# The second expert layer with its first product turned round, weights loaded for every tile, and another ending

## The chip, the cores and the metric

The kernel runs on one core of a Trainium2 chip. The metric is the device time of one execution in microseconds (us). A run of the profiler gives the trace of one execution, in which each engine's instructions stand with their starts and lengths.

## The reference

Three stages follow one another. All data are 32-bit floats.

```python
# 1: attention over 4 x 8 heads, 768 positions, 64 features: a band of +-15 keys, and block summaries of 32 keys
# 2: experts with a capacity: 3072 rows of 512, 8 experts with 384 rows each
h = np.maximum(x[mask] @ w1[e], 0.0);  out[mask] = h @ w2[e]
# 3: the second layer, on the rows of stage 2
out = x.copy()
do_compute = x @ w_skip > 0
xc = x[do_compute]
e_idx = np.argmax(xc @ w_gate, axis=1)         # gate_w: softmax weight of that expert
for e in range(8):                             # w1[e]: 512 x 1024, w2[e]: 1024 x 512
    h = np.maximum(xc[mask] @ w1[e], 0.0)
    y[mask] = gate_w[mask, None] * (h @ w2[e])
out[do_compute] = xc + y
```

How many rows each expert gets in the third stage depends on the data, so the kernel finds it out while it runs.

## The kernel before, in words

The attention fills the first part, the layer with capacities the middle. The change touches the third stage, from about 638 us, and what stands behind it.

The rows of the third stage are sorted by expert into **tiles of 128 rows** that share one expert. In this run there are 18 tiles. The first four (`KA = 4`) are made of the rows of the first six experts of stage 2, are laid out early and are unrolled in the program. The other 14 are made once all rows are known; their number stands in `ends_i` and is read by every engine with `tiles_in_use`. They run in a loop over `NSLOT = 32` slots, four slots a pass (two on ScalarE), and each slot stands behind a test `If(b < used)`.

What is done with one tile, engine by engine:

- **GpSimd** (POOL) fetches the 128 rows with `gather2` into one of four buffers `x2`, three tiles ahead; it waits for `o2_ready` of the tile, writes its result to `out` with `scatter2`, waits until that write has landed (`o2_out`), and tells VectorE so with `o2_written`.
- **TensorE** (PE) has `x2T`, the tile's rows transposed. `layer1` (line 1443) multiplies in two halves `h`: `x2T` is the stationary operand, 128 x 128 at a time, and 512 columns of `W1` stream past; four steps over the 512 features. Each such product of floats is two instructions in the trace, so this line has 16 a tile. The result has the rows of the tile on the partitions. ScalarE (ACT) writes it through a ReLU to `h2` (line 765). The second product needs `h2` the other way round, so `layer2` begins with eight transposes through PSUM (line 1454), which ScalarE copies to `h2T` (line 759). Between the two groups of four stand the four transposes of the next tile's rows (line 1433). Then eight products of 128 x 512, again 16 instructions, give `YB2` (line 1465).
- **VectorE** (DVE) multiplies by the gate and adds the row itself (`combine2`, line 1081).
- **SyncE** (SP) loads weights, 2 MB for `W1` (`load_w1`, line 397) and 2 MB for `W2` (`load_w2`, line 401), into two buffers each. For the first four tiles it loads both for each tile, into the buffer of its parity, once the tile two before has used it. After those it loads the weights of an expert once: experts 0 and 1, then the others that have tiles in the order of a list (`rank_i`, `list_i`) that VectorE works out in lines 1153 to 1163. It waits until each load has landed and raises `weights2_ready`. TensorE reads from `te_i` (lines 1166 to 1170) which expert a tile has, and takes its buffer as `r % 2`, an address that it computes.

The order on TensorE is the order of the program. In the unrolled part `totals2` stands behind tile 0, and `lists2` (line 1426: 24 products that give the token lists of the loop's tiles, 7 numbers for each of the `NSLOT` slots) between the two products of tile 2. `lists2` waits for `one_hots` on VectorE (lines 1055 to 1063). Then VectorE runs `combine2(0)`, the list of experts, `combine2(1)`, and `token_lists`.

The whole program is one `nc.Block()`. Where it ends each engine executes a drain, and they meet at a barrier.

Of the kernel before, what the change touches and what calls it, by code (L numbers as in the profile page):

```python
# [5 lines left out]
def banded_attention_two_moe_layers(nc, qT, kT, vwin, vblk, g1, w1a, w2a, skip2, g2, w1b, w2b, out):  # L6
    fp32, bf16, i32 = mybir.dt.float32, mybir.dt.bfloat16, mybir.dt.int32
    ALU = mybir.AluOpType
    ACT = mybir.ActivationFunctionType
# [31 lines left out]
    NSLOT = 32  # L41
# [18 lines left out]
    with ctx:  # L60
# [78 lines left out]
        def sba(name, shape, dt=fp32):  # L139
# [54 lines left out]
        with_w = sb("with_w", [128, E])  # L194
        rank = sb("rank", [128, E])
        rank_i = sb("rank_i", [128, E], i32)
        at_rank = sb("at_rank", [128, E, E])
        pick = sb("pick", [128, E, E])
        list_f = sb("list_f", [128, 2, E])
        list_i = sb("list_i", [128, 2, E], i32)  # L200
# [13 lines left out]
        h2 = sb("h2", [128, F])  # L214
# [12 lines left out]
        XB2, HT2, HB2, YB2 = bank[0], bank[1:3], bank[3:5], bank[5:7]  # L227
# [11 lines left out]
            gidx_now sidx_now x2_in0 x2_in1 x2_in2 x2_in3 x2_tr x2T_ready weights2_ready h2_mm h2_act h2_tr h2T_ready  # L239
            y2_mm o2_ready o2_out0 o2_out1 o2_written vec pool_c passed""".split()  # L240
# [5 lines left out]
        STARTED = """y_written y_st o2_written yT_ready h_act y_evac l2_evac h2_act h2T_ready o2_ready y2_mm""".split()  # L246
# [66 lines left out]
        block = ctx.enter_context(nc.Block())  # L313
# [3 lines left out]
        def _(sp):  # L317
# [99 lines left out]
            for e in range(2):  # L417
                sp.wait_ge(s["h2_mm"], 2 * (KA - 1 + e))
                load_w1(e, e)
                sp.wait_ge(s["y2_mm"], START + KA - 1 + e)  # L420
                load_w2(e, e)
                sp.wait_ge(s[f"w_in{e}"], 16 * ((E + KA) // 2 + 1))
                sp.wait_ge(s[f"w2_in{e}"], 16 * ((E + KA) // 2 + 1))
                sp.sem_inc(s["weights2_ready"], 1)
            sp.wait_ge(s["route2_ready"], 2)

            loaded = sp.value_load(rank_i[0:1, E - 1:E], min_val=2, max_val=E)
            for n in range(2, E):
                with sp.If(n < loaded):
                    last = sp.value_load(list_i[0:1, 1, n - 2:n - 1], min_val=0, max_val=NSLOT)  # L430
                    e = sp.value_load(list_i[0:1, 0, n:n + 1], min_val=0, max_val=E - 1)
                    wait(sp, "h2_mm", 2 * KA + 2 * last)
                    load_w1(e, n % 2)
                    wait(sp, "y2_mm", START + KA + last)
                    load_w2(e, n % 2)
                    sp.wait_ge(s[f"w_in{n % 2}"], 16 * ((E + KA) // 2 + n // 2 + 1))
                    sp.wait_ge(s[f"w2_in{n % 2}"], 16 * ((E + KA) // 2 + n // 2 + 1))
                    sp.sem_inc(s["weights2_ready"], 1)
# [3 lines left out]
        def _(pool):  # L442
# [177 lines left out]
            for b in range(KA):  # L620
# [7 lines left out]
                wait(pool, f"o2_out{b % 2}", 16 * (b // 2 + 1))  # L628
                pool.sem_inc(s["o2_written"], 1)
            pool.wait_ge(s["route2_ready"], 2)  # L630
            used = tiles_in_use(pool)
            with pool.Fori(0, NSLOT // NX) as i:
                for c in range(NX):
                    b = NX * i + c
                    with pool.If(b < used):

                        if c == 0:
                            wait(pool, "o2_ready", START + KA + b)
                        gather2(KA + b + NX - 1, (c + NX - 1) % NX)
                        wait(pool, "o2_ready", START + KA + b + 1)  # L640
                        scatter2(KA + b, c % 2)
                        wait(pool, f"o2_out{c % 2}", 16 * (KA // 2 + NX // 2 * i + c // 2 + 1))
                        pool.sem_inc(s["o2_written"], 1)
# [934 lines left out]
```

## Time and profile before

| | |
|---|---|
| time of three runs | 934.73, 937.4 and 938.68 us, median 937.4 |
| time of the profiled execution | 938.46 us, of which its span, first to last instruction, is 936.7 us |
| TensorE busy | 875.2 us, 93% of the span |
| VectorE, ScalarE, GpSimd busy | 470.7, 227.9 and 219.6 us |
| read from and written to HBM | 119.83 and 23.59 MB |
| weight loads of 2 MB | 38: 16 in the middle layer, 8 for the four unrolled tiles, 14 after them |
| granted TensorE clock | 0.98 of full speed on average |

PE is TensorE's matmul, PEld its weight load, which overlaps PE. A `q` behind an engine's name is its sequencer: registers, branches, semaphores and the issue of DMAs, which do not count as busy. The end of a matmul is modelled, so that one 512-column instruction is given as 593 ns while the next starts 429 ns after it. The distance of starts is what a stream of them costs. A line such as L1443 is a line of the kernel shown above.

### The profile page before, as it was taken

Reading aid. Unit: us, or ns where it says so; the run is one execution under the profiler, and the core shown is the slowest. Engines: PE = TensorE matmul, PEld = TensorE weight load, DVE = VectorE, ACT = ScalarE, POOL = GpSimd, SP = SyncE. Lnnn points to the kernel's source line nnn. Section 1 sums busy time; section 2 is a strip of 40 time slices with the busy share of each in tenths; the row PEclk is TensorE's granted clock in tenths of the full one; section 3 lists DMA queues with packets and bytes.
Section 4 is the critical chain, followed back from the end, with each engine's and each line's share of the span. In section 5 each row is a group of like instructions: output and inputs, shape, how many; then the busy total and the mean of one; then the engine's idle time right before and its main releaser. Section 6 shows DMA issues by size and latency. Waiting matters only on the chain.

```text
span 936.7 us, 14569 instructions
## 1 busy us (share of the span) xinstructions
PE 875.2 (93%) x4484; PEld 528.7 (56%) x4485; DVE 470.7 (50%) x2130; ACT 227.9 (24%) x698; POOL 219.6 (23%) x321
## 2 busy tenths in 40 slices
PE   4799999797899999999999999999999999999992
PEld 4689898785346454555546464645454444444441
DVE  8679886677776776767676763431810000000000
ACT  4456665321112020212111121212121212111120
POOL 3568874001020202012020202020021111112120
PEclk8899999899999999999999999999999999999997
DMA  7977751435060706143250607276778856033110
GB/s 205 269 207 222 217 164 41 156 143 186 27 232 23 258 23 218 63 171 111 91 189 13 246 23 257 87 266 229 261 264 295 294 203 212 34 123 115 34 34 4
DMA packets 58294, 145.39 MB, mean 155 GB/s; under 512 B 5841, under 2 KB 10449, under 8 KB 58241
## 3 DMA queue, kind: packets, MB, share of 16 engines
q1 hardware_dynamic: 43624, 114.63, 36.2%
q0 software_dynamic: 6960, 21.69, 6.9%
q10 hardware_dynamic: 7656, 8.36, 2.7%
q8 instruction: 33, 0.54, 0.2%
q14 instruction: 21, 0.16, 0.1%
HBM read 119.83 MB, written 23.59 MB: 153 GB/s over the span
## 4 chain that ended last, share of the span: by engine, by line
PE 78%; DVE 11%; DMA 4%; issue 3%; POOL 2%; ACT 0%; SPq 0%; DVEq 0%; POOLq 0%; ACTq 0%
PE bank L1320 15%; PE bank L1334 15%; PE bank L1465 14%; PE bank L1443 13%; DVE junk L925 3%; PE bank L1205 3%; PE bank L1227 3%; PE bank L1214 2%; PE bank L1490 2%; PE bank L1241 2%; PE bank L1454 2%; DMA vw<-vs 1%; PE bank L1393 1%; DMA kc<-in_kT 1%; PE bank L1482 1%
## 5 line engine op out<-in xcount | busy, mean ns | idle before, releaser
L1320 PE MATMUL bank<-xgT,W 128*128 128x384 f32 x512 | 179.9, 496 | 0.6 <-ACT xgT L694 0.6
L1334 PE MATMUL bank<-W,hT 128*128 128x512 f32 x384 | 178.8, 602 | 0.0
L925 DVE TENSOR_SCALAR_CACHE_REDUCE junk<-Vt,cand 128x192 bf16<-128x192 f32 x376 | 136.1, 410 | 4.8
L1465 PE MATMUL bank<-W,h2T 128*128 (+1 forms) x288 | 127.9, 597 | 0.2
L1443 PE MATMUL bank<-W,x2T 128*128 (+1 forms) x288 | 126.8, 593 | 0.0
L1081 DVE SCALAR_TENSOR_TENSOR o<-bank,gate,x 128x512 f32<-128x512 f32 x18 | 13.5, 750 | 225.2 <-PE bank L1465 225.1
L1320 PEld LDWEIGHTS bank<-xgT,W 128*128 128x128 f32 x512 | 90.6, 191 | 53.2 <-issue 3.6
L1334 PEld LDWEIGHTS bank<-W,hT 128*128 128x128 f32 x384 | 67.2, 191 | 57.9 <-issue 55.9
L1443 PEld LDWEIGHTS bank<-W,x2T 128*128 128x128 f32 x288 | 54.6, 191 | 67.3 <-issue 67.3
L1465 PEld LDWEIGHTS bank<-W,h2T 128*128 128x128 f32 x288 | 53.4, 190 | 63.8 <-issue 63.3
L659 ACT ACTIVATE pr<-bank,nmx 128x120 f32<-128x120 f32 x192 | 66.8, 365 | 37.7 <-DVE nmx L831 22.3
L765 ACT ACTIVATE h<-bank 128x512 f32<-128x512 f32 x36 | 21.5, 597 | 217.8 <-PE bank L1443 217.8
L699 ACT ACTIVATE hT<-bank 128x384 f32<-128x384 f32 x64 | 31.4, 490 | 150.1 <-PE bank L1320 150.1
L1205 PEld LDWEIGHTS bank<-kw,qz 128*128 128x128 f32 x384 | 55.6, 209 | 1.7
L484 POOL TENSOR_TENSOR pr<-pr,rinv 128x480 f32<-128x480 f32 x48 | 47.3, 985 | 36.2 <-DVE rinv L837 34.4
L1205 PE MATMUL bank<-kw,qz 128*128 128x120 f32 x384 | 55.2, 291 | 0.0
L288 POOL TENSOR_TENSOR hot_id<-hot,pnum 128x384 bf16<-128x384 f32 x7 | 8.2, 1167 | 188.1 <-DVE hot L989 188.1
L940 DVE TENSOR_SCALAR_CACHE_REDUCE reached<-bank 128x7 f32<-128x7 f32 x120 | 19.9, 166 | 61.7 <-PE bank L1393 61.7
L703 ACT ACTIVATE yb<-bank 128x512 f32<-128x512 f32 x24 | 14.3, 597 | 127.8 <-PE bank L1334 127.8
L570 POOL DMA_INDIRECT xg<-x_rows,gidx x24 | 23.6, 984 | 91.0 <-DVE gidx L905 86.1
L1227 PE MATMUL bank<-pT,vw 120*64 120x64 f32 x768 | 33.8, 232 | 11.8 <-issue 5.7
L577 POOL DMA_INDIRECT out<-yb,tok_i x24 | 23.7, 986 | 84.2 <-ACT yb L703 81.4
(277 smaller groups left out, 1108.5 us busy)
## 6 DMA issues: line engine op xcount, KB each, us to landing
W<-in_moe_w SPq DMA_DIRECT2D x38, 2048.0 KB, 8.7
vw<-in_vwin SPq DMA_DIRECT2D x16, 576.0 KB
qc<-in_qT SPq DMA_DIRECT2D x16, 384.0 KB, 6.5
kc<-in_kT SPq DMA_DIRECT2D x16, 384.0 KB, 7.6
vb<-in_vblk SPq DMA_DIRECT2D x16, 384.0 KB, 7.0
x_rows<-xr SPq DMA_DIRECT2D x24, 256.0 KB, 2.1
y_rows<-yb ACTq DMA_DIRECT2D x24, 256.0 KB, 2.0
vw<-vs ACTq DMA_DIRECT2D x14, 144.0 KB
```

The costliest lines, as they stand in the source:

```text
L484: g.tensor_tensor(pr[:, n % NP, :, :], pr[:, n % NP, :, :], rinv[:, n % NP, :].unsqueeze(2).to_broadcast([128, GW, KW]), ALU.mult) \
L570: g.indirect_dma_start(out=xg[:, j, :], out_offset=None, in_=x_rows, in_offset=bass.IndirectOffsetOnAxis(ap=gidx[:, j:j + 1], axis=0)) \
L577: g.indirect_dma_start(out=out, out_offset=bass.IndirectOffsetOnAxis(ap=tok_i[:, j:j + 1], axis=0), in_=yb[:, j, :], in_offset=None).then_ ...
L659: ins = a.activation(pr[:, n % NP, w, :], SC[n % 3][:, KW * w:KW * w + KW], ACT.Exp, scale=SCALE, bias=nmx[:, n % NP, w:w + 1], accum_out= ...
L699: a.activation(hT[:, r, :], HB[r % 2][:, 0:CAP], ACT.Relu).then_inc(s["h_act"], 1)
L925: ins = ve.tensor_scalar(junk[:, c, :], Vt[:, :], cand[:, c:c + 1].bitcast(fp32), 0.0, ALU.is_ge, ALU.add, accum_out=cnt[:, c:c + 1])
L1205: ins = mm(SC[n % 3][:, KW * w:KW * w + KW], qz[u % 2][:, GW * gr + w, :], kw[u % 2][:, GW * gr + w, :], start=False, stop=(w == GW - 1))
L1227: ins = mm(OB[n % 2][D * j:D * j + D, QW * w:QW * w + QW], vw[i][:, GW * gr + w, D * j:D * j + D], pT[:, n % 2, 128 * w + QW * j:128 * w + ...
L1320: ins = mm(HB[r % 2][:, 0:CAP], w1[:, c, 128 * r:128 * r + 128], xgT[:, c, :], start=(c == 0), stop=(c == KC - 1))
L1334: ins = mm(YB[j % 2][:, :], hT[:, r, 128 * j:128 * j + 128], w2[:, r, :], start=(r == 0), stop=(r == FC - 1))
L1443: ins = mm(HB2[h][:, :], x2T[par][:, c, :], W1[:, bass.ds(wb, 1), c * F + 512 * h:c * F + 512 * h + 512].rearrange("p o f -> p (o f)"), st ...
L1465: ins = mm(YB2[par][:, :], h2T[:, f, :], W2[:, bass.ds(wb, 1), f * DM:f * DM + DM].rearrange("p o f -> p (o f)"), start=(f == 0), stop=(f ...
```

## The change: what it does

- `layer1` takes 128 x 128 pieces of `W1` as the stationary operand and streams the 128 columns of `x2T`: eight pieces of 128 outputs with four steps each, 32 products. The result stands with the hidden features on the partitions. ScalarE writes it through the ReLU straight to `h2T`, and `h2`, its eight transposes and their two copies are gone.
- Each tile of the loop loads its own `W1` and `W2`, by the tile's parity, as the unrolled ones do. The list of experts is gone, `te_i` is computed earlier, before the slots, and has a semaphore of its own (`te_ready`). SyncE no longer waits for landings, and TensorE waits for the loads' own semaphores.
- `NSLOT` is 28. Every engine's loop tests once for a group of four (its first slot) and, inside, for each of the other three.
- GpSimd does not wait for each write of `out`. VectorE waits for the landing two tiles back itself; GpSimd waits once at the end for all of them, and for its gathers.
- The block is made with `no_gpsimd_drain=True`.

```diff
-    NSLOT = 32
+    NSLOT = 28
...
-        XB2, HT2, HB2, YB2 = bank[0], bank[1:3], bank[3:5], bank[5:7]
+        XB2, HB2, YB2 = bank[0], bank[3:5], bank[5:7]
...
-        block = ctx.enter_context(nc.Block())
+        block = ctx.enter_context(nc.Block(no_gpsimd_drain=True))
...
+            sp.wait_ge(s["te_ready"], 1)
+            used = tiles_in_use(sp)
+
+            def load_tile(i, c):
+                b = NX * i + c
+                e = sp.value_load(te_i[0:1, bass.ds(b, 1)], min_val=0, max_val=E - 1)
+                wait(sp, "h2_mm", 2 * (KA + b - 1))
+                load_w1(e, c % 2)
+                wait(sp, "y2_mm", START + KA + b - 1)
+                load_w2(e, c % 2)
+
+            with sp.Fori(0, NSLOT // NX) as i:
+                with sp.If(NX * i < used):
+                    load_tile(i, 0)
+                    for c in range(1, NX):
+                        with sp.If(NX * i + c < used):
+                            load_tile(i, c)
...
+            def turn(i, c):
+                b = NX * i + c
+                if c == 0:
+                    wait(pool, "o2_ready", START + KA + b)
+                gather2(KA + b + NX - 1, (c + NX - 1) % NX)
+                wait(pool, "o2_ready", START + KA + b + 1)
+                scatter2(KA + b, c % 2)
+
             with pool.Fori(0, NSLOT // NX) as i:
...
+                with pool.If(NX * i < used):
+                    turn(i, 0)
+                    for c in range(1, NX):
+                        with pool.If(NX * i + c < used):
+                            turn(i, c)
+            wait(pool, "o2_out0", 16 * ((used + KA + 1) // 2))
+            wait(pool, "o2_out1", 16 * ((used + KA) // 2))
+            for buf in range(NX):
+                wait(pool, f"x2_in{buf}", 16 * ((used + KA + 2 * NX - 2 - buf) // NX))
...
             def hidden2(b, par):
                 for h in range(2):
                     act.wait_ge(s["h2_mm"], 2 * b + h + 1)
-                    a.activation(h2[:, 512 * h:512 * h + 512], HB2[h][:, :], ACT.Relu).then_inc(s["h2_act"], 1)
-                h2T_evac(b, 0)
+                    a.activation(h2T[:, 4 * h:4 * h + 4, :], HB2[h][:, :].rearrange("p (c t) -> p c t", c=4), ACT.Relu) \
+                        .then_inc(s["h2_act"], 1)
                 x2T_evac(b + 1, 1 - par, XB2)
-                h2T_evac(b, 1)
...
-            def combine2(b, par, buf):
+            def combine2(b, par, buf, written):
                 dve.wait_ge(s["y2_mm"], START + b + 1)
-                dve.wait_ge(s["o2_written"], START + b - 1)
+                if not isinstance(b, int) or b >= 2:
+                    dve.wait_ge(s[f"o2_out{par}"], 16 * written)
...
+            te = [128, NSLOT, E]
+            o.step(ve.tensor_tensor(te_c[:, :, :], bc(iotaS[:, :], te, 2), bc(ends[:, :], te, 1), ALU.is_ge))
+            o.step(ve.tensor_reduce(te_f[:, :], te_c[:, :, :], X, ALU.add))
+            o.step(ve.tensor_scalar(te_f[:, :], te_f[:, :], float(E - 1), None, ALU.min))
+            ve.tensor_copy(te_i[:, :], te_f[:, :]).then_inc(s["te_ready"], 1)
...
                 pe.wait_ge(s["h2_act"], START + 2 * b + h - 1)
-                for c in range(KC):
-                    ins = mm(HB2[h][:, :], x2T[par][:, c, :],
-                             W1[:, bass.ds(wb, 1), c * F + 512 * h:c * F + 512 * h + 512].rearrange("p o f -> p (o f)"),
-                             start=(c == 0), stop=(c == KC - 1))
+                for c in range(4):
+                    at = 512 * h + 128 * c
+                    for k in range(KC):
+                        ins = mm(HB2[h][:, 128 * c:128 * c + 128], W1[:, par, k * F + at:k * F + at + 128], x2T[par][:, k, :],
+                                 start=(k == 0), stop=(k == KC - 1))
                 ins.then_inc(s["h2_mm"], 1)
...
-            def layer2(b, par, wb, next_buf, next_uses):
-                for h in range(2):
-                    pe.wait_ge(s["h2_act"], START + 2 * b + h + 1)
-                    if h == 0:
-                        pe.wait_ge(s["h2T_ready"], START + 2 * b)
-                    for c in range(4):
-                        ins = tr(HT2[h][:, 128 * c:128 * c + 128], h2[:, 128 * (4 * h + c):128 * (4 * h + c) + 128],
-                                 ident[:, :])
-                    ins.then_inc(s["h2_tr"], 1)
-                    if h == 0:
-                        x2_transpose(b + 1, next_buf, next_uses, XB2)
+            def layer2(b, par, uses, next_buf, next_uses):
+                x2_transpose(b + 1, next_buf, next_uses, XB2)
                 pe.wait_ge(s["o2_ready"], START + b - 1)
-                if isinstance(b, int):
-                    pe.wait_ge(s[f"w2_in{wb}"], 16 * (E // 2 + b // 2 + 1))
+                pe.wait_ge(s[f"w2_in{par}"], 16 * (E // 2 + uses))
                 for f in range(FC):
                     if f % 4 == 0:
-                        pe.wait_ge(s["h2T_ready"], START + 2 * b + f // 4 + 1)
+                        pe.wait_ge(s["h2_act"], START + 2 * b + f // 4 + 1)
```

## Rows read from the trace of the kernel before

**Rows 1.** The page: busy us, share of the span and instructions of each engine.

```profile
PE 875.2 (93%) x4484; PEld 528.7 (56%) x4485; DVE 470.7 (50%) x2130; ACT 227.9 (24%) x698; POOL 219.6 (23%) x321
```

**Rows 2.** Stretches: length, busy PE, PEld, DVE, ACT, POOL, clock, DMA share, GB/s.

```profile
704.93:919.57 214.64, 214.43 (x617) 102.85 (x615) 10.51 (x14) 37.27 (x70) 33.16 (x56) 1.00 0.40 142
919.57:936.70 17.13, 0.00 (x0) 0.00 (x0) 0.75 (x1) 0.00 (x0) 1.19 (x2) 0.61 0.01 2
```

**Rows 3.** The chain that ended last, through one tile: start, us, what.

```profile
704.93 6.87 PE bank L1443 x16
711.80 0.44 PE bank L1454 x4
...
712.67 0.47 PE bank L1454 x4
...
713.16 7.11 PE bank L1465 x16
```

**Rows 4.** The chain again, where 128-column products of another line stand together.

```profile
641.85 0.89 PE bank L1490 x8
...
643.18 1.84 PE bank L1490 x16
```

**Rows 5.** The attention's products of 120 columns: timeline, then ns of one (min/median/max).

```profile
150.29 1.05 PE L1205 MATMUL bank<-kw,qz 128*128 128x120 f32 x8
```

```profile
L1205 PE MATMUL bank<-kw,qz x8: 268/276/276, 150.3 to 151.1; 128*128 128x120 f32 x8
```

**Rows 6.** ScalarE's second ReLU of that tile, and the sequencer's next slot test.

```profile
711.84 0.60 ACT L765 ACTIVATE h<-bank 128x512 f32<-128x512 f32 x1 [2.84 <-PE bank L1443]
```

```profile
L1539 PEldq COMPARE_BRANCH  x1: 68/68/68, 714.5 to 714.5; - x1
```

**Rows 7.** VectorE's first and last one-hots, one `te` step, and `lists2`.

```profile
665.09 0.96 DVE L1055 TENSOR_TENSOR oneB<-mx,iotaS 128x768 bf16<-128x768 f32 x1
...
672.49 3.99 DVE L1063 TENSOR_SCALAR oneA<-iota_bf,slot 128x128 bf16<-128x128 bf16 x24
...
680.46 0.42 DVE L1168 TENSOR_REDUCE te_f<-te_c 128x32 f32<-128x256 f32 x1
```

```profile
679.07 2.30 PE bank L1426 x24
```

**Rows 8.** Landings of all 11 `W2` loads, and columns as in Rows 2.

```profile
DMA to landing us min/median/max: 8.3/10.2/12.9
```

```profile
700.00:715.00 15.00, 14.98 (x45) 7.23 (x44) 0.75 (x1) 2.66 (x5) 2.37 (x4) 1.00 0.86 315
```

**Rows 9.** Two weight loads issued together, and the landing of the second.

```profile
749.78 0.37 SPq L397 DMA_DIRECT2D W<-in_moe_w  x1
751.07 0.37 SPq L401 DMA_DIRECT2D W<-in_moe_w  x1
```

```profile
DMA to landing us min/median/max: 12.1/12.1/12.1
```

**Rows 10.** DMA queues of 704.9 to 766.2 us (q8) and of 766.3 to 919.6 (all).

```profile
q8 instruction: 2, 0.03, 0.2%
```

```profile
q1 hardware_dynamic: 3136, 8.39, 15.5%
q0 software_dynamic: 1600, 4.84, 9.3%
```

**Rows 11.** The last tile's result and its write: start, us, engine, line.

```profile
919.78 0.75 DVE L1081 SCALAR_TENSOR_TENSOR o<-bank,gate,x 128x512 f32<-128x512 f32 x1 [14.58 <-PE bank L1465]
...
921.85 1.01 POOL L610 DMA_INDIRECT out<-o,now_s  x1 [0.90 <-POOL now_s L608]
```

**Rows 12.** GpSimd's sequencer after 920 us: waits, slot tests, drain (count, ns, first and last start).

```profile
L278 POOLq EVENT_SEMAPHORE  x3: 17/17/17, 920.6 to 924.1; - x3
```

```profile
L635 POOLq COMPARE_BRANCH  x18: 45/45/50, 924.4 to 929.0; - x18
```

```profile
L60 POOLq DRAIN  x1: 7187/7187/7187, 929.3 to 929.3; - x1
```

More of the change, by code:

```diff
@@ L238, in banded_attention_two_moe_layers @@
             gate_sub gate_exp rows8_ready base8_mm teA_ready onehot2_ready id2_mm gid2_ready route2_ready
-            gidx_now sidx_now x2_in0 x2_in1 x2_in2 x2_in3 x2_tr x2T_ready weights2_ready h2_mm h2_act h2_tr h2T_ready
-            y2_mm o2_ready o2_out0 o2_out1 o2_written vec pool_c passed""".split()
+            gidx_now sidx_now x2_in0 x2_in1 x2_in2 x2_in3 x2_tr x2T_ready te_ready h2_mm h2_act
+            y2_mm o2_ready o2_out0 o2_out1 vec pool_c passed""".split()
         s = {n: sem(n) for n in names}
         START = 1
-        STARTED = """y_written y_st o2_written yT_ready h_act y_evac l2_evac h2_act h2T_ready o2_ready y2_mm""".split()
+        STARTED = """y_written y_st yT_ready h_act y_evac l2_evac h2_act o2_ready y2_mm""".split()
         class Order:
@@ L416, in _ @@
                 load_w2(e, k % 2)
[L417 to L438, printed above, removed]
+            sp.wait_ge(s["te_ready"], 1)
[13 more added lines that the diff above has]
+                            load_tile(i, c)
         @block.gpsimd
@@ L773, in _ @@
                 hidden2(b, b % 2)
-            act.wait_ge(s["route2_ready"], 2)
+            act.wait_ge(s["te_ready"], 1)
             used = tiles_in_use(act)
-            with act.Fori(0, NSLOT // 2) as i:
-                for par in range(2):
-                    with act.If(2 * i + par < used):
-                        hidden2(KA + 2 * i + par, par)
+            with act.Fori(0, NSLOT // NX) as i:
+                with act.If(NX * i < used):
+                    hidden2(KA + NX * i, 0)
+                    for c in range(1, NX):
+                        with act.If(NX * i + c < used):
+                            hidden2(KA + NX * i + c, c % 2)
         @block.vector
@@ L1150, in _ @@
             one_hots(NT, NSLOT)
[L1151 to L1171 removed]
+            combine2(0, 0, 0, 0)
+            combine2(1, 1, 1, 0)
             dve.wait_ge(s["id2_mm"], 2)
@@ L1174, in _ @@
             for b in range(2, KA):
-                combine2(b, b % 2, b % NX)
+                combine2(b, b % 2, b % NX, b // 2)
             dve.wait_ge(s["route2_ready"], 2)
@@ L1179, in _ @@
             with dve.Fori(0, NSLOT // NX) as i:
-                for c in range(NX):
-                    b, par = NX * i + c, c % 2
-                    with dve.If(b < used):
-                        combine2(KA + b, par, c)
+                with dve.If(NX * i < used):
+                    combine2(KA + NX * i, 0, 0, KA // 2 + NX // 2 * i)
+                    for c in range(1, NX):
+                        with dve.If(NX * i + c < used):
+                            combine2(KA + NX * i + c, c % 2, c, KA // 2 + NX // 2 * i + c // 2)
         @block.tensor
```

84 lines of the change are left out of this document (19 added, 65 removed).

## The prediction, on record before the changed kernel ran

> **What bounds the kernel now.** I read the page first, for the share of each engine, then busy time by stretch, then the chain that ended last, and at the end the sequencers' own records. TensorE is busy for 93% of the span [rows 1]. In the loop of the second layer it is busy for 214.43 of 214.64 us at the full granted clock, while VectorE has 10.5, ScalarE 37.3 and GpSimd 33.2 us, and the DMA engines are at 0.40 [rows 2]. So in this loop only what TensorE executes costs time: 214.64 us for 14 tiles are 15.33 us a tile. The chain shows the parts of a tile: 6.87 us for the first product, 0.44 + 0.44 + 0.47 for transposes (the middle group, line 1433, is as long as the first), a short rest, and 7.11 us for the second product up to the next tile [rows 3]. Behind the last product come 17.13 us in which TensorE does nothing [rows 2]. There the chain goes through VectorE's last result at 919.78 and GpSimd's write issued at 921.85, and then through nothing that counts as busy [rows 11]. GpSimd's sequencer shows what it is: the write has landed at 924.1, 18 slots are tested until 929.3, and a drain takes 7.19 us [rows 12]. It ends at 936.5, 0.2 us before the span does. These are two places with different limits, and the change touches both.
>
> **The first product.** It is 16 instructions of 512 columns in 6.87 us, 0.429 each [rows 3]. It becomes 64 of 128 columns (32 products, two instructions each), each with a weight load of its own. The columns streamed are the same, 8192; the question is what a short one costs more. The nearest rows are another line with the same shape and kind, also accumulating in fours: 8 in 0.89 us and 16 in 1.84, that is 0.111 and 0.115 each [rows 4]. With them a tile's 64 take 7.12 to 7.36 us. I take 0.1115, so 7.14, because the 16 hold one stop of some 0.05 us at a semaphore wait. That is +0.27 a tile. The weight load is hidden in these rows, as it is for 512 columns.
>
> The Trainium skill (TensorE: Matmul & The Clock Gate, "LDWEIGHTS (loading the stationary operand)") puts a load of 128 columns at P / 1.2, 107 ns, whatever the matmul. The trace fits this as a floor: products of only 120 columns are no closer than (1.05 - 0.28) / 7 = 0.11 us, the last one's modelled length of 0.276 taken off [rows 5]. If load and product ran one after the other, 64 x 0.214 would be 13.7 us a tile and the kernel some 120 us slower. Rows 4 speak against it, since they hold both in 0.111.
>
> **The transposes.** Eight go, 0.44 + 0.47 us [rows 3]. The chain's first transpose starts at 711.80, the second product's instructions at 713.16, and by the chain the three groups take 1.35 us of these 1.36. The second group and the first products behind it cost more than the bare 8 x 0.109: 0.47 against 0.44, and 7.11 against 16 x 0.429 = 6.87. The reason I read is that the sequencer has to stop at a late event: the second ReLU runs from 711.84 to 712.44 [rows 6], and the second four transposes wait for it, so the sequencer's lead is used up and each further wait shows. In the new order nothing near waits for a late event. The second product's first half needs the first ReLU, which ends some 3 us before; its second half needs the second ReLU 0.8 us after the first product's end, and gets to it only after 0.44 + 8 x 0.43 = 3.9 us. Elsewhere the sequencer runs far ahead: it tests the next slot at 714.5, 5.7 us before TensorE is done with the tile [rows 6]. So I expect 7.14 + 0.44 + 6.87 = 14.45, and 0.10 for waits that still show: **14.55 us a tile**, 0.78 less than 15.33. Bounds: 14.44 with no stop at all, and 14.9 if products cost 0.115 (+0.22) and the stop of 0.24 in the second product stays in part.
>
> For 18 tiles (the four unrolled ones have the same parts) this is 18 x 0.78 = 14.0 us. `lists2` streams 196 instead of 224 columns: 2.30 us x 1/8 = 0.3 less [rows 7]. Together TensorE ends **14.3 us** earlier, between 8 and 16.
>
> **What must stay hidden.** `one_hots` is ready at 676.5 and `lists2` begins at 679.07, so it has 2.6 us [rows 7]. Moving four `te` steps ahead of it adds about 0.45 + 0.45 + 0.2 + 0.2 = 1.3 us, and 28 slots instead of 32 take an eighth off the 7.4 us from 665.09 to 672.49, 0.9. TensorE comes there 1.2 us sooner (two tiles' saving, less one longer first product). That leaves about 1 us: cost nothing, 0.5 at the worst. The list's eleven steps and the late `te_i` go from VectorE, which waits there anyway. ScalarE loses two copies of 0.6 us a tile and is idle most of the time. GpSimd's gathers run three tiles ahead and no longer stand behind a landing; the landing that VectorE now waits for itself was issued two tiles, 29 us, before.
>
> **Weights for every tile.** 14 tiles x 2 loads of 2.10 MB replace 14 loads: 14 x 2.10 = 29 MB more. Demand is 4.19 MB of weights, 0.26 MB gathered and 0.26 MB written a tile: 4.72 MB in 14.55 us, 324 GB/s. Before, where each tile loaded its own, 315 GB/s took 0.86 of the DMA engines [rows 8], so 324 takes 0.89. The room in time is larger: a load is issued when the tile two before is done with the buffer, and is needed 7.0 + 14.5 = 21.5 us later. It lands 8.3 to 12.9 us after its issue [rows 8]. Issued almost together, two landed within 751.07 + 12.1 - 749.78 = 13.4 us, below a tile's time even if pairs didn't overlap [rows 9]. SyncE waits for `h2_mm` and `y2_mm` in the order in which they come, and nothing else is queued on it. Cost 0; without that cover it is the difference of 4.72 MB's transfer and 14.55 us, times 14 (below).
>
> **The end.** Before: 17.15 us from TensorE's end to the span's. The write's issue ends 3.29 us after TensorE (922.86) and stays [rows 11]. Then GpSimd walks on without waiting for the landing: 18 tests and their loop ends took 5.2 us before [rows 12], 0.29 each; now two tests remain in the group of the last tile and one for each of three groups, with more loop ends per test, about 2.2 us. The landing (1.3 us) is under it. Then six waits on values worked out from `used`. No row shows them. Between nothing and 4.5 us; 0.11 us for a register step (about 46 in those 5.2 us) and three or four steps a wait give 2.3, which I take. The drain's 7.19 us go, the barrier's 0.2 to 0.3 stays. In sum 3.3 + 2.2 + 2.3 + 0.3 = 8.1 us in place of 17.15: **9.0 us less**, between 6.7 and 12.2 (the landing alone then sets the end).
>
> **Sum.** 14.3 + 9.0 = 23.3 us off the profiled 938.46 gives 915.2. That execution lay 1.06 above the median of 937.4, so **914 us**; with the bounds 909 to 923.
>
> **Rivals.**
> 1. *The drain's work is paid elsewhere*, by whatever follows the last instruction in the 1.76 us outside the span, or by GpSimd in another instruction. For it: the drain took 7.19 us although its last write had landed 5 us before, so it isn't that write. Against: no other engine waits for it except at the barrier. 914 + 7.2 = 921 us.
> 2. *Short products starve the sequencer* or the stops stay: 128 instructions in 7.1 us are one each 56 ns, and the waits stand between short ones. For it: the one stop in rows 4. Against: in the 8 of the same row 0.111 holds, with a load each. A tile then takes 15.2 us and TensorE gains next to nothing; only the end pays: 914 + 18 x 0.65 = 926.
> 3. *Weights starve the tiles*, the slower side. If loads on SyncE's queue do not overlap, two of the median 10.2 us [rows 8] make 20.4 us a tile: 914 + 14 x 5.85 = 996. It begins to cost at 14.55 us for 4.72 MB, and makes the kernel slower than 942 from 16.55 us on, 285 GB/s. Rows 8 and 9 speak against it; for it, that so far at most seven tiles in a row loaded, and with pauses.
> 4. *Instructions for the loop are fetched anew.* Four tiles were 352 weight loads and products and are now 672. In the first pass the instruction queue moved two packets, and later nothing [rows 10]: the old loop stayed in the engine. If the new one does not, each jump stops the sequencer. A price from rows: a packet of about 1 us and a landing of 2 to 4 us as for other transfers, say 3 us, less what is queued. Three jumps between passes give 9 us, and three skipped groups with two jumps each 18 us behind the last product, in place of 8 us on GpSimd: about 20 us back, 934.
>
> The Trainium skill (Runtime: NRT & Kernel Launch, "Instruction fetch mechanics") gives TensorE room for 2048 instructions, which would hold this loop, but also says that a taken branch outside the two pages at hand stops for a fetch. By the first the sum is unchanged, by the second rival 4 holds; rows 10 show only that the smaller loop stayed.
>
> **Chances.** Forecast 0.73; rival 1 0.07; rival 2 0.07; rival 3 0.07; rival 4 0.06. A measurement of this kernel tells 0.5%, 4.7 us, from no change. Forecast, rivals 1 and 2 are faster; rival 4 I split between faster and the same; rival 3 is mostly slower. That makes 0.88 faster, 0.05 the same, 0.07 slower. The range 908 to 924 holds the forecast with the bounds and rival 1, 0.8 together.
>
> **What would show it.** TensorE's line of the first product in 64 instructions, 7.1 us in the chain; 14.5 us between tiles; no idle time of PE by a DMA; DMA share near 0.9 through the whole loop; no instruction packets after the loop's first pass; from the last product to the end about 8 us and no long drain. I am wrong if tiles are 15 us or more apart, if the first product waits for `W`, or if the time outside the span grows by the drain.

## The result, and the profile after

The changed kernel takes 913.66 us (median of four runs, 909.39 to 915.92) where the kernel before takes 937.95 (four runs beside them, 934.73 to 938.68). The ratio is 0.974, with a 95% interval of 0.970 to 0.979. That is 24.3 us less; 23.3 off the profiled execution had been predicted. The profiled execution took 909.39 us, 907.6 of it span, and is itself the fastest of the four.

The page, busy time and instructions of each engine; its counterpart is [rows 1].

```profile
PE 860.7 (95%) x5204; PEld 587.5 (65%) x5204; DVE 467.2 (51%) x2118; ACT 210.4 (23%) x662; POOL 219.9 (24%) x321
```

Stretches of the kernel after, columns as in [rows 2]: from the second layer's first product to the start of the loop, from there to the last product's end, and the rest. The last line is the part of the loop in which weights are loaded without a break.

```profile
636.58:699.74 63.16, 63.16 (x392) 47.75 (x392) 24.26 (x90) 8.73 (x17) 8.12 (x13) 1.00 0.83 292
699.74:902.05 202.31, 202.30 (x1176) 148.37 (x1175) 10.51 (x14) 23.55 (x42) 33.46 (x56) 1.00 0.81 294
902.05:907.60 5.55, 0.00 (x0) 0.00 (x0) 0.75 (x1) 0.00 (x0) 1.19 (x2) 0.98 0.02 6
```

```profile
720.00:865.00 145.00, 145.00 (x847) 106.73 (x846) 7.51 (x10) 16.82 (x30) 23.92 (x40) 1.00 0.89 321
```

The loop's 14 tiles went from 214.64 to 202.31 us, at the same full clock and with TensorE still without a gap; the DMA share doubled from 0.40 to 0.81, and TensorE waits for none of it. The 0.81 is an average over the whole loop, and for its last two tiles nothing is left to load; while loads run, the share is 0.89 at 321 GB/s, what the prediction worked out (0.89, 324). The last stretch went from 17.13 to 5.55 us. The whole second layer, first product to last, took 281.16 us before (638.41 to 919.57) and takes 265.47 now (636.58 to 902.05). So the change gave **15.7 + 11.6 = 27.3 us** in this pair of traces. The span differs by 29.1, because this execution also reached the second layer 1.8 us sooner. I do not count that part as an effect of the change: times of one and the same kernel differ by more (by 9 us in number 1; see the last section).

The chain that ended last, through one tile of the loop (start, us, what), and through `lists2`, beside [rows 3] and [rows 7].

```profile
699.74 7.14 PE bank L1421 x64
706.88 0.44 PE bank L1410 x4
707.32 6.87 PE bank L1432 x16
714.19 7.14 PE bank L1421 x64
```

```profile
675.94 2.04 PE bank L1403 x24
```

A tile is 714.19 - 699.74 = 14.45 us, in every one of the 15 intervals behind `lists2` (from one second product to the next), and it holds nothing but its three groups: 64 short products at 0.1115, four transposes, 16 long products at 0.429. Before it was 15.33 in the loop. The unrolled tiles of the kernel before were a little shorter, which [rows 3] do not show. The fourth, with nothing of `lists2` in it, took 704.93 - 689.69 = 15.24 us, and its chain has a shorter second product:

```profile
697.43 0.47 PE bank L1454 x4
697.90 7.03 PE bank L1465 x16
```

The timeline of the end (start, us, engine, line), beside [rows 11], and GpSimd's sequencer there (count, ns, first and last start), beside [rows 12].

```profile
902.19 0.75 DVE L1070 SCALAR_TENSOR_TENSOR o<-bank,gate,x 128x512 f32<-128x512 f32 x1 [13.59 <-PE bank L1432]
903.18 0.18 POOL L595 COPY now_s<-sidx 128x1 int32 x1 [10.20 <-DVE o L1070]
904.26 1.01 POOL L597 DMA_INDIRECT out<-o,now_s  x1 [0.90 <-POOL now_s L595]
```

```profile
L626 POOLq COMPARE_BRANCH  x4: 48/53/53, 904.5 to 905.9; - x4
L269 POOLq FUSED_REGOPS  x6: 73/73/100, 906.0 to 907.2; - x6
L60 POOLq EVENT_SEMAPHORE  x2: 17/17/17, 907.4 to 907.5; - x2
```

Instead of 18 slot tests there are four, over by 906.0; the six final waits take until 907.3, and the second of them ends with the landing of the last write; there is no drain on GpSimd. The landing, and the event that ends that wait, from the same trace:

```profile
DMA to landing us min/median/max: 2.3/2.3/2.3
L270 POOLq EVENT_SEMAPHORE  x1: 17/17/17, 906.5 to 906.5; - x1
```

The write has landed at 904.26 + 2.3, about 906.5. The time outside the span is 909.39 - 907.6 = 1.8 us, as before (1.76).

### The profile page after: what moved, and what is told of

It reads as the page before. It is cut to its first block, busy times and chain, and to the rows that moved or that the text cites. A ratio compares the mean times of both kernels' runs of the same rounds, so it can differ in the third digit from the quotient of the medians.

```text
span 907.6 us, 15611 instructions
## 1 busy us (share of the span) xinstructions
PE 860.7 (95%) x5204; PEld 587.5 (65%) x5204; DVE 467.2 (51%) x2118; ACT 210.4 (23%) x662; POOL 219.9 (24%) x321
## 4 chain that ended last, share of the span: by engine, by line
PE 78%; DVE 12%; DMA 5%; issue 3%; POOL 2%; ACT 1%; SPq 0%; DVEq 0%; POOLq 0%; ACTq 0%
PE bank L1297 15%; PE bank L1311 15%; PE bank L1421 14%; PE bank L1432 14%; DVE junk L913 3%; PE bank L1182 3%; PE bank L1204 3%; PE bank L1191 2%; PE bank L1455 2%; DMA vw<-vs 2%; PE bank L1218 2%; PE bank L1370 1%; DMA kc<-in_kT 1%; PE bank L1447 1%; PE bank L1286 1%
## 5 line engine op out<-in xcount | busy, mean ns | idle before, releaser
L1421 PEld LDWEIGHTS bank<-x2T,W 128*128 128x128 f32 x1152 | 131.4, 192 | 7.7 <-issue 7.7
L1421 PE MATMUL bank<-x2T,W 128*128 128x128 f32 x1152 | 131.8, 275 | 0.0
L1432 PE MATMUL bank<-W,h2T 128*128 128x512 f32 x288 | 126.6, 592 | 0.0
L752 ACT ACTIVATE h2T<-bank 128x512 f32<-128x512 f32 x36 | 21.5, 597 | 220.0 <-PE bank L1421 220.0
L595 POOL COPY now_s<-sidx 128x1 int32 (+1 forms) x18 | 3.3, 183 | 193.3 <-DVE o L1070 193.3
L1370 PEld LDWEIGHTS bank<-cnt,same_e 128*128 128x128 bf16 x136 | 13.2, 97 | 50.7 <-DVE junk L913 45.1
```

The source lines that it names most:

```text
L1421: ins = mm(HB2[h][:, 128 * c:128 * c + 128], W1[:, par, k * F + at:k * F + at + 128], x2T[par][:, k, :], start=(k == 0), stop=(k == KC - 1))
L1432: ins = mm(YB2[par][:, :], h2T[:, f, :], W2[:, par, f * DM:f * DM + DM], start=(f == 0), stop=(f == FC - 1))
```

## The experiments

All start from the changed kernel. Times are medians, ratios are to the kernel before on the same chip (937.7 us beside the first four, 936.7 beside the next four, 939.9 beside the last three). For the end I count from the start of VectorE's last result, which is on every trace: 16.92 us before, 5.41 after.

### 1. The drain put back

```diff
-        block = ctx.enter_context(nc.Block(no_gpsimd_drain=True))
+        block = ctx.enter_context(nc.Block())
```

> The changed kernel with the drain of GpSimd put back, nothing else. Theory (the drain is 7.2 us of waiting that only the end pays): the span ends in a drain of about 7.19 us on GpSimd, from the last product to the end 5.55 + 7.2 = 12.7 us, the time rises by 7.2 to about 921 us. Rival (its work is paid by whatever follows when it is left out): the span grows by 7.2 us but the time outside the span shrinks, and the time stays near 914. Tiles stay 14.45 us apart under both.

Measured 915.6 us (six runs, 913.3 to 922.3), ratio 0.977 (0.973 to 0.981). GpSimd's sequencer:

```profile
L60 POOLq DRAIN  x1: 7187/7187/7187, 904.9 to 904.9; - x1
```

VectorE's last result starts at 899.61 and the span ends at 912.3: 12.7 us, 7.3 more than after. The profiled execution took 914.04, 1.7 outside its span. So the drain is paid in full when it is there and nowhere when it isn't. Medians of separate executions show less of it (915.6 against 913.7 and, in a later pair, 910.3) since they scatter by some us for another reason; the stretch settles it.

### 2. Light loads

```diff
-                load_w1(e, c % 2)
+                sp.dma_start(W1[:, c % 2, 0:F], w1b[bass.ds(e, 1), 0:128, :].rearrange("o p f -> p (o f)")).then_inc(s[f"w_in{c % 2}"], 16)
...
-                load_w2(e, c % 2)
+                sp.dma_start(W2[:, c % 2, 0:DM], w2b[bass.ds(e, 1), 0:128, :].rearrange("o p f -> p (o f)")).then_inc(s[f"w2_in{c % 2}"], 16)
```

The loop loads a quarter of `W1` and an eighth of `W2`; the rest of the buffers keeps older weights, so most of the loop's results come from other weights.

> The changed kernel, but each tile of the loop loads only the first quarter of its W1 and the first eighth of its W2 (0.79 MB in place of 4.19), so that the loop's results are computed from other weights. Theory (the loads lie wholly beside the products): tiles still 14.45 us apart, time the same, 914 us within 3. Rival (the 29 MB more cost something that does not show as a wait, by slower reads of the operands): tiles closer than 14.45, and up to some us less in all.

Measured 910.7 us (909.4 to 915.2), ratio 0.972 (0.967 to 0.976); tiles 14.45. The median is 3.3 us under the 914 that both texts started from, but the changed kernel itself came out at 910.35 in number 11. The stretch from 720 to 890 us, columns as above:

```profile
720.00:890.00 170.00, 170.00 (x980) 124.08 (x979) 9.01 (x12) 19.59 (x35) 26.50 (x46) 1.00 0.27 83
```

With 83 GB/s in place of 309 (the changed kernel over the same stretch) not one tile is faster. The loads cost nothing, neither by waits nor by slowing what TensorE reads.

### 3. The old first product and its transposes

The first product again with 512 columns, and h's transposes and ScalarE's two copies back (they too as in the kernel before), with per-tile loads and the new end kept. The buffer of the weights is then still `par`, a constant, and not `wb`, read from a register.

```diff
-                for c in range(4):
-                    at = 512 * h + 128 * c
-                    for k in range(KC):
-                        ins = mm(HB2[h][:, 128 * c:128 * c + 128], W1[:, par, k * F + at:k * F + at + 128], x2T[par][:, k, :],
-                                 start=(k == 0), stop=(k == KC - 1))
+                for c in range(KC):
+                    ins = mm(HB2[h][:, :], x2T[par][:, c, :], W1[:, par, c * F + 512 * h:c * F + 512 * h + 512],
+                             start=(c == 0), stop=(c == KC - 1))
...
-                x2_transpose(b + 1, next_buf, next_uses, XB2)
+                for h in range(2):
+                    pe.wait_ge(s["h2_act"], START + 2 * b + h + 1)
+                    if h == 0:
+                        pe.wait_ge(s["h2T_ready"], START + 2 * b)
+                    for c in range(4):
+                        ins = tr(HT2[h][:, 128 * c:128 * c + 128], h2[:, 128 * (4 * h + c):128 * (4 * h + c) + 128],
+                                 ident[:, :])
+                    ins.then_inc(s["h2_tr"], 1)
+                    if h == 0:
+                        x2_transpose(b + 1, next_buf, next_uses, XB2)
```

> The changed kernel with the old first product, its eight transposes and the copies of them; the loads for every tile, the slots and the ending stay changed. Theory (the product and its transposes are worth 0.88 us a tile and nothing else in the loop is): tiles 15.33 us apart, 18 x 0.88 = 15.8 us more than the changed kernel, about 929.5 us; the end still 5.6 us. Rival (a part of the 0.88 is from buffers whose address no longer comes from a register): tiles at 15.1 to 15.2, 926 us.

Measured 926.7 us (925.2 to 927.7), ratio 0.987 (0.983 to 0.991); the end as after (5.4 us), tiles 15.24. The chain through one tile:

```profile
752.58 6.87 PE bank L1426 x16
759.45 0.44 PE bank L1436 x4
759.88 0.44 PE bank L1417 x4
760.32 0.47 PE bank L1436 x4
760.79 7.03 PE bank L1446 x16
```

So the rival came true: of the 0.88 us a tile, the product's form with its transposes is 15.24 - 14.45 = 0.79. The other 0.09 sits at the start of the second product (7.03 here, 7.11 before) and came with the per-tile loads. What differs there is the weights' address, a constant here and out of a register before. The kernel before bears this out: its fourth unrolled tile has constant addresses too, and the same 7.03 and 15.24. In its loop TensorE's sequencer executes register steps among the second product's instructions, and neither number 3 nor the unrolled tile has any there:

```profile
L1465 PEldq ALU_OP  x5: 32/32/32, 713.1 to 713.9; - x5
```

The first of them stands between the wait for ScalarE's copy and the first weight load, which starts 0.21 us behind the copy's end; here it starts 0.11 behind it. A kernel with only the addresses changed, and the new product in the old kernel, weren't tried.

### 4. Single slot tests and 32 slots

```diff
-    NSLOT = 28
+    NSLOT = 32
...
-                with pool.If(NX * i < used):
-                    turn(i, 0)
-                    for c in range(1, NX):
-                        with pool.If(NX * i + c < used):
-                            turn(i, c)
+                for c in range(NX):
+                    with pool.If(NX * i + c < used):
+                        turn(i, c)
```

> The changed kernel with 32 slots again, and GpSimd testing each slot by itself. Theory: 18 tests and loop ends in 5.2 us start where the last write is issued, then the six waits, 1.4 us; the end is 904.26 + 5.2 + 1.4 + 0.2 = 911.0 in place of 907.6, 3.5 us more behind the last product, plus 0.3 us for lists2 with 32 slots: 917.5 us. Rival (the tests hide under the landing of the write): the same time as the changed kernel.

Measured 915.3 us (909.2 to 920.6), ratio 0.977 (0.972 to 0.982). GpSimd's sequencer:

```profile
L628 POOLq COMPARE_BRANCH  x18: 45/45/50, 901.0 to 905.7; - x18
```

From VectorE's last result (899.12) to the span's end 8.3 us, 2.9 more than after; the tile with `lists2` is 0.26 us longer (16.75 between second products against 16.49). The first test comes at 901.0, before the write's issue (901.20 to 902.21): GpSimd's sequencer walks on while the issue runs. 2.9 is less than the 3.5 expected, in part because the tests start so early, and in part because the write lands at 903.5, long before the six waits, which take 1.2 us here and 1.35 in the changed kernel. The medians (915.3 and 913.7) lie too close for their scatter to tell anything.

### 5 and 6. More to load

A third load on SyncE for every tile, into a buffer that nothing reads: 1.05 MB, then 1.57 MB (`0:6 * 128`). SyncE also waits for its landing one tile on.

```diff
+            def load_extra(e):
+                sp.dma_start(hT[:, :, :].rearrange("p r t -> p (r t)")[:, 0:4 * DM].rearrange("p (c f) -> p c f", c=4),
+                             w2b[bass.ds(e, 1), 0:4 * 128, :].rearrange("o (c p) f -> p (o c) f", p=128)).then_inc(s["extra_in"], 16)
...
                 load_w2(e, c % 2)
+                wait(sp, "extra_in", 16 * (b + 1))
+                load_extra(e)
```

> The changed kernel with a third load for each tile of the loop, 1.05 MB into a buffer that nobody reads. 5.77 MB a tile in 14.45 us are 399 GB/s, about what the engines moved when they were full (412 GB/s at a share of 1.04). Theory (the weights are hidden and the limit is the rate when full, about 400): tiles 14.45 us apart still, or up to 0.3 more. Rival (the limit is near what the loop needs already, 330 GB/s): 5.77 MB take 17.5 us a tile, 40 us more in all.

> The same with 1.57 MB more for each tile, 6.29 MB. Theory: the DMA engines set the pace now, 6.29 MB / 400 GB/s = 15.7 us a tile, and the first product waits for its weights; 14 x 1.27 = about 15 to 18 us more than the changed kernel, some 930 us. Rival (330 GB/s): 19 us a tile, 60 us more.

With 1.05 MB: 909.4 us (two runs, 908.3 and 910.5), tiles 14.45. With 1.57 MB: 920.6 (918.9 and 922.4), ratio 0.982 (0.977 to 0.987); the first seven intervals behind `lists2` are 14.45, the eighth is 14.61, and the last seven are 15.15 to 15.98, most of them near 15.9. The same stretch of both, the smaller load first:

```profile
720.00:890.00 170.00, 170.00 (x980) 124.09 (x979) 9.01 (x12) 19.59 (x35) 27.06 (x46) 1.00 1.02 388
```

```profile
720.00:890.00 170.00, 163.70 (x945) 118.59 (x944) 8.26 (x11) 19.60 (x35) 26.28 (x44) 1.00 1.04 396
```

And the weights' issues in that stretch (count, KB each, median us to landing), the changed kernel, then the two in the same order, and TensorE's waits in the last one (us in total, times, longest).

```profile
W<-in_moe_w SPq DMA_DIRECT2D x22, 2048.0 KB, 8.0
```

```profile
W<-in_moe_w SPq DMA_DIRECT2D x22, 2048.0 KB, 11.7
```

```profile
W<-in_moe_w SPq DMA_DIRECT2D x22, 2048.0 KB, 18.4
PE bank L1430 <- DMA W<-in_moe_w: 6.3, 6, 1.3
```

Starved tiles, rival 3, are thereby a mechanism that exists, with its point: 4.72 + 1.57 = 6.29 MB in 15.87 us are 396 GB/s, and that is what this mix of transfers reaches. Its other version, loads that do not overlap, is out: in number 5 they land 11.7 us after their issue, and two are issued every 14.45 us. The queue first eats the room in time (landing 11.7 us after issue with no tile late, 18.4 in number 6, against the 21.5 us there are), and then tiles wait. In number 6 SyncE also stands 88.6 us, in 14 waits, for the extra load before it can issue the next `W1`, so some of the room goes there; the share stays at 1.04 meanwhile, so the rate is the limit all the same. The tiles are as long as expected (15.7), but the time is not: 11 us more than number 5, where 15 to 18 over the changed kernel were expected, since only the last seven intervals are late by more than 0.2. By that rate the changed kernel's 4.72 MB need 11.9 of its 14.45 us. The Trainium skill (HBM Reference, "Specifications (TRN2)") gives a core about 358 GB/s when both cores of a pair stream and about 425 when one streams alone; 396 on this one core is above the first and below the second, and no run here shows a pair.

### 7 and 8. Eight transposes that nobody needs

Eight transposes of the identity a tile into the two free banks, four before x's transposes and four behind; in the second kernel the last four also wait for the second ReLU, as the old ones did.

```diff
+            def spare(b, par, h):
+                for c in range(4):
+                    tr(bank[1 + h][:, 128 * c:128 * c + 128], ident[:, :], ident[:, :])
...
+                spare(b, par, 0)
                 x2_transpose(b + 1, next_buf, next_uses, XB2)
+                pe.wait_ge(s["h2_act"], START + 2 * b + 2)
+                spare(b, par, 1)
```

The `wait_ge` is in the second kernel only.

> The changed kernel with eight transposes a tile put back at their old places, of the identity into a bank that nobody reads, without a wait of their own. Theory (0.109 each, and the rest of the old tile's time was the stop at the second ReLU): tiles 14.45 + 0.87 = 15.32 us apart. Rival (the stops come with each short group whatever it waits for): 15.5.

> The same, and the second four wait for the tile's second ReLU, as the old ones did. Theory (the wait for a late event takes the sequencer's lead, and the waits behind it then show): 0.15 to 0.25 us more than without the wait, 15.5 us a tile. Rival (the wait is met in time and costs nothing): the same 15.32.

One execution each: 928.2 us with tiles of 15.32, and 925.8 with tiles of 15.36. (The first is the longer in all because it reached the second layer 3.1 us later, 639.53 against 636.46.) The chain of the first, then of the second:

```profile
759.46 0.44 PE bank L1427 x4
759.89 0.44 PE bank L1410 x4
760.33 0.44 PE bank L1427 x4
760.77 6.87 PE bank L1438 x16
```

```profile
757.46 0.47 PE bank L1427 x4
757.93 6.87 PE bank L1439 x16
```

Transposes cost 0.87 us for eight, as the sum had them. But the wait for the second ReLU, which I had made the source of the stops, adds 0.03 us to the transposes behind it (0.04 to the tile, where 0.15 to 0.25 were expected) and leaves the second product at its bare 6.87. I had put the old 7.11 down to the wrong wait.

### 9. A shorter end

GpSimd copies the last tile's row numbers before it waits for `o2_ready`, with a wait for the landing two tiles back that makes that safe, and at the very end waits for its gathers ahead of its writes.

```diff
+                wait(pool, "o2_ready", START + b + 1)
...
-                wait(pool, "o2_ready", START + KA + b + 1)
+                wait(pool, f"o2_out{c % 2}", 16 * (KA // 2 + NX // 2 * i + c // 2))
```

> The changed kernel with two steps of GpSimd moved: a tile's row numbers are copied before the wait for its result, not behind it, and at the end the four waits for gathers stand before the two for the last writes. Theory: the copy and its wait (0.43 us of the 1.29 between the wait for the result and the last write's issue) go, and four waits of 0.2 us hide under the landing; from the last product to the end 5.1 in place of 5.7 us, 0.6 us off the time, which the runs can't tell from nothing. Rival (something else ends last, such as the landing itself): 5.5 or more.

Measured 910.4 us (six runs, 907.5 to 913.7), ratio 0.970 (0.967 to 0.973). Timeline of the end:

```profile
900.85 0.75 DVE L1072 SCALAR_TENSOR_TENSOR o<-bank,gate,x 128x512 f32<-128x512 f32 x1 [13.59 <-PE bank L1434]
902.49 1.00 POOL L598 DMA_INDIRECT out<-o,now_s  x1 [11.09 <-DVE o L1072]
```

The write is issued 1.64 us after VectorE's start instead of 2.07, and the end is 905.7 - 900.85 = 4.8 us instead of 5.4. Of the 0.6 us, 0.43 is the copy's; the other 0.2 is the landing, which held the second of the six final waits in the changed kernel and comes before the waits for the writes here. In the median it can't be told from number 11.

### 10. A cover for ScalarE's copy

Number 3 with four transposes of the identity (`tr(bank[7]...)`) ahead of the second product's waits, in the loop only. If the second product stops because ScalarE's first copy of h's transposes ends late, they fill the stop and cost less than their own 0.44 us.

> The kernel with the old first product (tiles 15.24 us apart in the loop) and, in the loop, four more transposes of the identity behind the old second group, before the waits of the second product. Theory (the old order lost about 0.15 us a tile because the second product waits for ScalarE's first copy, which ends when the second group is issued): the four cover it, and tiles are 15.24 + 0.44 - 0.15 = 15.53 us apart. Rival (the stop is that of any waits between short instructions): 15.24 + 0.44 = 15.68.

One execution, 931.1 us; tiles 15.52 against 15.24, so 0.28 more for 0.44 us of work. The chain:

```profile
745.28 0.47 PE bank L1436 x4
745.75 0.44 PE bank L1442 x4
746.19 6.87 PE bank L1448 x16
```

The second product is at 6.87 again. In the kernel before, the two things stand side by side in the timeline, the copy on ScalarE and the weight load of the product that reads it:

```profile
712.33 0.59 ACT L759 ACTIVATE h2T<-bank 128x512 f32<-128x512 f32 x1
...
713.13 0.30 PEld L1465 LDWEIGHTS bank<-W,h2T 128*128 128x128 f32 x2 [0.23 <-issue]
```

The copy ends at 712.92 and the load starts at 713.13, while a transpose starts every 0.11 us before it: the load waits for the copy (and, in the loop of the kernel before, for the register step of number 3). With the cover the stop is gone: 0.16 us a tile.

### 11. The changed kernel again

> The changed kernel once more, beside the run of e9 on the same chip. Theory: the stretch from the second layer's first product to the last is 265.45 us as in its first profile, and the end 5.7; the start of that stretch is where executions differ (633 to 640 us in the profiles so far); the median of the times about 913, 24.5 us below the kernel before. Rival (something behind the second layer's start varies too): another length of the stretch.

Measured 910.35 us (six runs, 908.7 to 912.6), ratio 0.969 (0.966 to 0.972), tiles 14.45, end 5.4. From the start of the second layer's first product to the end of its last it has the same length as the first trace, to 0.01 us. Neither this nor number 9 beats the other beyond its scatter; number 9 is the best end by its stretch, 0.6 us.

## Why the prediction was right

**What bounds the loop** was right: everything that TensorE executes there costs its own time, and nothing else costs any but the stops of the old order, 0.27 us a tile (below). Number 7 adds 0.87 us of work and the tile grows by 0.87; number 2 takes three quarters of the traffic away and nothing moves.

**The first product.** 0.1115 for one of 128 columns with its own weight load, from another line with the same shape [rows 4], gave 7.14 us; measured 7.14. Rival 2 is out.

**The transposes.** 0.87 us for eight were right (number 7). The stops were in the old trace as I sized them (15.33 - 6.87 - 3 x 0.44 - 6.87 = 0.27) and are all gone: the tile is the lower bound, 14.45, and not 14.55. The term "0.10 for waits that still show" was mis-sized; it measured nothing. And the cause I gave was only a small part: the second ReLU costs 0.04 (number 8), ScalarE's first copy 0.16 (number 10), the register's address 0.09 (number 3 and the unrolled tiles of the kernel before). The sum did not rest on the cause: it added up the bare groups of the new order, and the change took away all three stops at once, two of which I had not seen. With 0.27 for the dearer product the account of a tile is 0.87 + 0.04 + 0.16 + 0.09 - 0.27 = 0.89, measured 0.88. Had the copies stayed and only the ReLU's wait gone, my reading would have promised a gain that doesn't come.

**TensorE in all.** Predicted 14.3 us (18 x 0.78 + 0.3), measured 15.7; the bounds were 8 and 16. The 0.88 holds for the 14 tiles of the loop only, 12.3 us. The prediction took the four unrolled ones to have the same parts; they had no register addresses to lose and gave between 0.72 and 0.80 each, 3.1 us, and `lists2` gave 0.26 (2.30 to 2.04).

**What must stay hidden** did: VectorE's last `one_hots` row ends at 670.31 + 4.00 = 674.31, and `lists2` begins at 675.94, 1.6 us later, where I had left about 1. Weights for every tile cost 0 as said, in rate (321 GB/s against a limit of 396) and in time (8.0 us to landing of 21.5). Rival 3 begins where a tile moves 396 GB/s x 14.45 us = 5.7 MB, a fifth more than it does; number 5, with 4.72 + 1.05 = 5.77, stands just at that point.

**Instructions.** In the loop's first pass (699 to 757.5 us) the instruction queue moved three packets, and behind it, from 757.6 to 902, it doesn't appear; the queues there:

```profile
q1 hardware_dynamic: 13595, 35.68, 68.6%
q0 software_dynamic: 1600, 4.84, 8.4%
issues: line engine op xcount, KB each, median us to landing
```

The loop of 672 loads and products stayed in the engine as the one of 352 did, and no tile at a jump is longer than the others. Rival 4 is out, and of the Trainium skill's two statements (Runtime: NRT & Kernel Launch, "Instruction fetch mechanics") the trace agrees with the room for 2048 instructions, not with a fetch at a taken branch. A jump back does cost the sequencer more than a branch that falls through (0.07 us), but only 0.22 us, and it was 0.22 in the kernel before too; it lies under products already queued:

```profile
L1500 PEldq COMPARE_BRANCH  x3: 221/221/237, 751.0 to 866.6; - x3
```

**The end.** Predicted 8.1 us in place of 17.15, measured 5.55 in place of 17.13: two terms were mis-sized, both too high. In the terms of the sum, 3.3 + 2.2 + 2.3 + 0.3, the trace has 3.2 + 0.7 + 1.35 + 0.3. I laid GpSimd's walk through the slots behind the write's issue, which ends at 905.27; but its four tests begin at 904.5, while the issue runs, and the walk is over at 906.0, 0.7 us behind the issue (number 4 shows the same with 18 tests). And the six waits took 1.35 us (906.0 to 907.34), not 2.3: each is one register step of 0.07 to 0.1 and a wait, 0.2 us in all, where I had counted three or four steps of 0.11. The landing does not lie wholly under the walk, as I had said: at 906.5 it ends the second wait 0.2 us late, and number 9, whose waits for the gathers come first, saves that. The drain's term was right: 7.19 us predicted, 7.3 measured between number 1 and the changed kernel, and the time outside the span is 1.8 with and without it. Rival 1 is out.

**The sum.** The terms that the change moved give 27.3 us, 4.0 more than the 23.3 predicted (1.4 in the tiles, 2.6 in the end). The medians taken beside each other differ by 24.3 us in the result and by 29.5 in number 11 (939.88 and 910.35), on either side of 27.3. The first four executions' 913.7 agrees with my 914 better than the terms do; this closeness is partly luck of those executions.

## What to carry to other kernels

Where one engine has no gap, price a change by that engine's own instructions from rows of the same shape elsewhere in the trace, and look for what each dropped operation had behind it: here eight transposes took with them two copies on another engine and a stop of 0.16 us a tile that no view names as a wait, only as a group that is longer than its count of products. Reloading data that could be kept costs nothing until the transfers' rate or their room in time is used up; measure that point with a load that nobody needs, and look at the landing, which lengthens (8.0 to 11.7 us in number 5) before anything waits. At a program's end count what each sequencer still has to walk through, and let it overlap with the last transfer.

## What the runs showed of the hardware

The queue behind the loads gives no warning in TensorE's time: at a DMA share of 1.02 and 388 GB/s not one tile is late (number 5), and 0.5 MB more a tile makes most of the last seven 1.4 us longer, after seven of the loop's tiles on credit (number 6).

TensorE's sequencer was far ahead at the end. It reached the block's end at 898.7 and stood in its drain for 3.4 us until the products were done:

```profile
L60 PEldq DRAIN  x1: 3410/3410/3410, 898.7 to 898.7; - x1
```

In the kernel before the same drain took 0.008 us, with TensorE's slot tests still to walk behind its last products. That a wait for a late event costs by using up this lead is my reading; no run varies the lead.

Executions reach the second layer between 633.1 us (number 4) and 640.4 (number 3), though the code until there is nearly the same in all. With this goes how long TensorE's clock is granted at 1.2 and not at 2.4 GHz, above all in the attention's first 60 us. The first stretch of number 4 and of number 3 (the clock is the third number from the end):

```profile
0.00:60.00 60.00, 44.56 (x427) 40.64 (x428) 46.59 (x109) 29.77 (x133) 34.94 (x58) 0.89 0.84 241
```

```profile
0.00:60.00 60.00, 40.93 (x363) 37.22 (x363) 41.55 (x98) 27.59 (x122) 30.45 (x52) 0.83 0.82 224
```

At 0.89 TensorE has done 427 products by then, at 0.83 it has done 363. Up to 190 us the mean is 0.96 of full speed in number 4 and 0.92 in number 3, which is 190 x 0.04 = 7.6 us of full clock, about the 7.3 us that they lie apart. Over all the traces the late ones are mostly those with more time at the lower clock, but not strictly (number 1 has 0.91 in its first 60 us and is 0.7 us later than number 4), and why it is granted longer in some is open. It is why medians of the same kernel came out at 913.7 and 910.35, and why differences under some 5 us were read from stretches here and not from medians.
